# First down product of the second layer placed inside the third pair's products, with part of the first z's way back issued by ScalarE

## What is computed

```
x: 3072 x 512 (output of the first layer), w_in: 512 x 1024, w_out: 1024 x 512
h   = x @ w_in
e   = exp(h - max(h)) ;  solu = h * e / (sum(e) + 1e-9)
z   = (solu - mean(solu)) / sqrt(var(solu) + 1e-6) * g_ln
out = z @ w_out
```

## Time and profile before

| | us |
|---|---|
| median of 3 runs | 869.15 (868.05 to 872.74) |
| profiled execution | 869.12 |
| its span (first to last instruction) | 867.3 |
| outside the span | 1.82 |
| TensorE busy | 857.2 (99%) |
| VectorE / ScalarE / GpSimd busy | 449.7 (52%) / 332.3 (38%) / 241.0 (28%) |
| mean granted TensorE clock | 0.998 of full |

### The profile page before, as it was taken

One profiled execution on the slowest core, in us unless ns is written; L12 is line 12 of the kernel. 1 busy time (PEld: TensorE's weight loads), 2 busy tenths in 40 slices (PEclk: granted clock), 3 DMA queues, 4 the chain that ended last, 5 costly groups with the idle time before them and its releaser, 6 DMA issues.

```text
span 867.3 us, 12108 instructions
## 1 busy us (share of the span) xinstructions
PE 857.2 (99%) x4816; PEld 700.5 (81%) x4816; DVE 449.7 (52%) x770; ACT 332.3 (38%) x505; POOL 241.0 (28%) x228
## 2 busy tenths in 40 slices
PE   8999999999999999999999999999989999999998
PEld 7788878888888888888888788888868888888886
DVE  5545543333433333323432333567889899898831
ACT  2433342122311233112321223256456667676542
POOL 2654543222232222222222122227411111221000
PEclk9999999999999999999999999999999999999999
DMA  9921102111111111121021104300155654446451
GB/s 335 370 76 59 49 21 78 49 50 49 49 60 51 49 37 61 49 71 52 0 85 37 37 1 143 101 25 24 43 170 184 176 176 153 146 152 191 130 165 66
DMA packets 50744, 82.85 MB, mean 96 GB/s; under 512 B 5248, under 2 KB 23680, under 8 KB 50688
## 3 DMA queue, kind: packets, MB, share of 16 engines
q1 hardware_dynamic: 50688, 82.08, 29.0%
HBM read 56.90 MB, written 25.17 MB: 95 GB/s over the span
## 4 chain that ended last, share of the span: by engine, by line
PE 97%; DMA 1%; DVE 1%; SPq 1%; ACT 0%; issue 0%; DVEq 0%
PE acc L413 31%; PE h L383 29%; PE o_ps L947 15%; PE p L887 13%; PE att L320 3%; PE att L331 2%; PE att L355 1%; PE att L345 1%; DMA q<-in_q 1%; PE acc L331 0%; DMA zt<-z 0%; PE h L400 0%; SPq L219 0%; DVE x_lo L603 0%; SPq L852 0%
## 5 line engine op out<-in xcount | busy, mean ns | idle before, releaser
L413 PE MATMUL acc<-g_hi,w 128*128 128x512 f32 x768 | 257.2, 396 | 0.0
L383 PE MATMUL h<-x_hi,w 128*128 128x512 f32 x760 | 249.8, 389 | 0.5 <-DVE x_lo L603 0.5
L734 POOL TENSOR_TENSOR g_lo<-g_raw,g_hi 128x512 fp32r<-128x512 f32 x96 | 126.2, 1315 | 396.2 <-ACT g_hi L454 396.2
L506 ACT ACTIVATE g_raw<-g_raw,half_bias 128x512 f32<-128x512 f32 x96 | 69.5, 724 | 337.1 <-DVE g_raw L662 337.1
L413 PEld LDWEIGHTS acc<-g_hi,w 128*128 128x128 f32 x768 | 144.1, 188 | 35.1 <-issue 3.4
L383 PEld LDWEIGHTS h<-x_hi,w 128*128 128x128 f32 x760 | 142.7, 188 | 30.6 <-DVE x_lo L603 0.9
L662 DVE TENSOR_SCALAR g_raw<-h 128x512 f32<-128x512 f32 x96 | 66.2, 690 | 172.2 <-PE acc L413 172.2
L413 PE MATMUL acc<-g_lo,w 128*128 128x512 f32 x384 | 149.6, 390 | 0.0
L383 PE MATMUL h<-x_lo,w 128*128 128x512 f32 x380 | 147.9, 389 | 0.0
L667 DVE TENSOR_TENSOR g_raw<-h,g_raw 128x512 f32<-128x512 f32 x96 | 66.4, 692 | 69.6 <-ACT g_raw L506 69.6
L454 ACT ACTIVATE g_hi<-g_raw 128x512 fp32r<-128x512 f32 x96 | 60.7, 632 | 72.8 <-DVE g_raw L667 72.8
(11 more groups left out here) (116 smaller groups left out, 1051.9 us busy)
## 6 DMA issues: line engine op xcount, KB each, us to landing
z<-zq SPq DMA_DIRECT2D x24, 512.0 KB, 2.7
zt<-z SPq DMA_DIRECT2D x96, 128.0 KB, 3.1
kT<-in_kT SPq DMA_DIRECT2D x24, 256.0 KB, 2.7
q<-in_q SPq DMA_DIRECT2D x24, 256.0 KB, 2.6
v<-in_v SPq DMA_DIRECT2D x24, 256.0 KB, 3.0
x2T<-y SPq DMA_DIRECT2D x24, 256.0 KB, 2.6
x_raw<-x2T SPq DMA_DIRECT2D x12, 512.0 KB, 4.8
out<-o SPq DMA_DIRECT2D x24, 256.0 KB, 4.4
```

The costliest lines, as they stand in the source:

```text
L383: last = mm(hb[f % 2][:, :], ww, xx[:, kt, :], start=kt == 0 and t == 0, stop=kt == KT - 1 and t == 2)
L413: last = mm(acc[m][:, :], ww, gg[:, f % 2, :], start=f == 0 and t == 0, stop=f == FT1 - 1 and t == 2)
L506: nc.scalar.activation(gate[:, f % 2, :], gate[:, f % 2, :], ACT.Square, bias=half_bias[:, 0:1], scale=0.5).then_inc(sem["squared"], 1)
L734: tt(g[1][:, f % 2, :], gate[:, f % 2, :], g[0][:, f % 2, :].bitcast(F32), ALU.subtract)\
```

## The change

- TensorE: `down(0)` no longer follows `up(1)`. In `up(2)` the order of the products becomes 1, 4, `down(0)`, 2, 6, 7, 5, 3; the other pairs keep 1, 2, 6, 7, 4, 5, 3. The waits on `products` are counted through `done(n, product)`.
- ScalarE: `output(0)` moves from the end of round 1 to round 2, behind `split_z(2)`. In round 1, behind `copy_part(1)`, ScalarE waits for the stored first z (`zq_stored[0]`) and issues two of the four loads of `get_z(0)`.
- SyncE: `get_z(0)` issues only the first two loads. `store(0)` moves from round 2, where it was ahead of `put_z(4)`, to the end of round 2, behind `get_z(5)`.
- VectorE: `turn_squares(0, SECOND)` goes ahead of `bias(0, FIRST)`; `split_z(0)` goes behind `join_p5(1)` and `join_p3(1)`.

```diff
-    DOWNS = {1: (0,), 2: (1, 2), 3: (3, 4), 4: (5,), 5: (6, 7), 6: (8, 9), 7: (10,), 8: (11, 12), 9: (13, 14),
+    ORDER = (1, 2, 6, 7, 4, 5, 3)
+    THIRD = (1, 4, 2, 6, 7, 5, 3)
+
+    DOWNS = {2: (1, 2), 3: (3, 4), 4: (5,), 5: (6, 7), 6: (8, 9), 7: (10,), 8: (11, 12), 9: (13, 14),
              10: (15,)}
...
+        def done(n, product):
+            return 7 * n + (THIRD if n == 2 else ORDER).index(product) + 1
+
+        def quarter(s, q):
+            squares = z_dram[s % 2].rearrange("(i r) (q x) -> q r i x", r=SQ, q=P // SQ)
+            return zt[q * SQ:(q + 1) * SQ, s % 2, :, :, :].rearrange("r i f c -> r i (f c)"), squares[q]
...
-                squares = z_dram[s % 2].rearrange("(i r) (q x) -> q r i x", r=SQ, q=P // SQ)
-                for q in range(P // SQ):
-                    sp.dma_start(zt[q * SQ:(q + 1) * SQ, s % 2, :, :, :].rearrange("r i f c -> r i (f c)"),
-                                 squares[q]).then_inc(sem["zt_loaded"][s % 2], 16)
+                for q in range(2 if s == 0 else P // SQ):
+                    dst, src = quarter(s, q)
+                    sp.dma_start(dst, src).then_inc(sem["zt_loaded"][s % 2], 16)
 
             for n in range(PAIRS2 - 1):
                 if n + 2 < PAIRS2:
                     load_x2(n + 2)
-                for s in DOWNS.get(n - 1, ()):
-                    store(s)
+                if n >= 3:
+                    for s in DOWNS[n - 1]:
+                        store(s)
                 put_z(2 * n)
                 put_z(2 * n + 1)
                 get_z(2 * n)
                 get_z(2 * n + 1)
                 if n == 0:
                     finish["store_x2"]()
+                if n == 2:
+                    store(0)
...
+                def p4():
+                    wait(pe, sem["taken"], 5 * n - 1)
+                    product(bank_of(n, 4), a(1, SECOND), t(2))
...
+                def p3():
+                    pe.wait_ge(sem["taken"], 5 * n + (1 if n else 3))
+                    product(bank_of(n, 3), s(3), b(1, RIGHT))
...
+                elif n == 2:
+                    p1()
+                    p4()
+                    down(0)
+                    p2()
+                    p6()
+                    p7()
+                    p5()
+                    p3()
...
             for n in range(1, PAIRS2 - 2):
                 copy_part(n)
+                if n == 1:
+                    act.wait_ge(sem["zq_stored"][0], 16)
+                    act.wait_ge(sem["g_used"], BLOCKS * FT1 - 1)
+                    for q in range(2, P // SQ):
+                        dst, src = quarter(0, q)
+                        nc.scalar.dma_start(dst, src).then_inc(sem["zt_loaded"][0], 16)
                 split_x(n + 1)
                 split_z(2 * n - 2)
+                if n == 2:
+                    output(0)
...
-                for s in DOWNS[n]:
+                for s in DOWNS.get(n, ()):
                     output(s)
...
             variance(0, FIRST)
+            turn_squares(0, SECOND)
             bias(0, FIRST)
-            turn_squares(0, SECOND)
             finish["dve_evacuate"]()
             turn_squares(0, FIRST)
...
             join_p7(1)
             join_p4(1)
-            split_z(0)
             join_p5(1)
             join_p3(1)
+            split_z(0)
             split_x(2, True)
```

More of the change, by code:

```diff
@@ L902, in t, with p1, p2, p6 @@
                     return [lambda k, w=w: w[:, i, k, :] for w in w_sum]
+                def p1():
+                    wait(pe, sem["part_copied"], n)
+                    pe.wait_ge(sem["x2_lo"], 2 * n + 1)
+                    product(bank_of(n, 1), a(0, FIRST), b(0, LEFT))
+                def p2():
+                    wait(pe, sem["h_max"], 2 * n)
+                    product(bank_of(n, 2), a(1, FIRST), b(1, LEFT))
+                def p6():
+                    pe.wait_ge(sem["x2_lo"], 2 * n + 2)
+                    product(bank_of(n, 6), s(1), t(1))
+                def p7():
+                    product(bank_of(n, 7), s(2), b(0, RIGHT))
+                def p4():
+                    wait(pe, sem["taken"], 5 * n - 1)
+                    product(bank_of(n, 4), a(1, SECOND), t(2))
+                def p5():
+                    product(bank_of(n, 5), s(0), t(0))
+                def p3():
+                    pe.wait_ge(sem["taken"], 5 * n + (1 if n else 3))
+                    product(bank_of(n, 3), s(3), b(1, RIGHT))
                 if n == 0:
@@ L908, in up @@
                     pe.wait_ge(sem["w2_in_lo"], 7)
[L909 to L916, removed]
+                    p1()
+                    p2()
                     pe.wait_ge(sem["gmax"], BLOCKS * FT1 - 1)
-                pe.wait_ge(sem["x2_lo"], 2 * n + 2)
-                product(bank_of(n, 6), s(1), t(1))
-                if n == 0:
+                    p6()
                     pe.wait_ge(sem["part_copied"], 1)
[L922 to L925, removed]
+                    p7()
                     finish["pe_down"](FT1 - LAG - 1)
@@ L928, in up @@
                     pe.wait_ge(sem["taken"], 1)
-                if n == 1:
+                    p4()
+                    pe.wait_ge(sem["taken"], 2)
+                    p5()
+                    p3()
+                elif n == 1:
+                    pe.wait_ge(sem["h_max"], 2)
+                    p1()
+                    p2()
+                    p6()
+                    pe.wait_ge(sem["gmax"], BLOCKS * FT1)
+                    p7()
                     for par in range(2):
                         pe.wait_ge(sem["acc_free"][par], 2 * BLOCKS)
[L932 to L937, removed]
+                    p4()
+                    p5()
+                    p3()
+                elif n == 2:
+                    p1()
+                    p4()
+                    down(0)
+                    p2()
+                    p6()
+                    p7()
+                    p5()
+                    p3()
+                else:
+                    p1()
+                    p2()
+                    p6()
+                    p7()
+                    p4()
+                    p5()
+                    p3()
             def down(s):
@@ L973, in copy_part @@
             def copy_part(n):
-                act.wait_ge(sem["products"], 7 * n + 1)
+                act.wait_ge(sem["products"], done(n, 1))
                 wait(act, sem["h_max"], 2 * n)
@@ L1089, in join_p2 @@
                 dve.wait_ge(sem["part_copied"], n + 1)
-                dve.wait_ge(sem["products"], 7 * n + 2)
+                dve.wait_ge(sem["products"], done(n, 2))
                 add_with_maximum(h2[:, FIRST, LEFT], bank_of(n, 2)[:, :], part, -3.4e38, st("h_first", FIRST))\
@@ L1094, in join_p6 @@
             def join_p6(n):
-                dve.wait_ge(sem["products"], 7 * n + 3)
+                dve.wait_ge(sem["products"], done(n, 6))
                 dve.wait_ge(sem["taken"], 5 * n + 1)
@@ L1099, in join_p7 @@
             def join_p7(n):
-                dve.wait_ge(sem["products"], 7 * n + 4)
+                dve.wait_ge(sem["products"], done(n, 7))
                 dve.wait_ge(sem["taken"], 5 * n + 2)
@@ L1104, in join_p4 @@
             def join_p4(n):
-                dve.wait_ge(sem["products"], 7 * n + 5)
+                dve.wait_ge(sem["products"], done(n, 4))
                 dve.wait_ge(sem["taken"], 5 * n + 3)
@@ L1110, in join_p5 @@
             def join_p5(n):
-                dve.wait_ge(sem["products"], 7 * n + 6)
+                dve.wait_ge(sem["products"], done(n, 5))
                 dve.wait_ge(sem["taken"], 5 * n + 4)
@@ L1118, in join_p3 @@
             def join_p3(n):
-                dve.wait_ge(sem["products"], 7 * n + 7)
+                dve.wait_ge(sem["products"], done(n, 3))
                 dve.wait_ge(sem["taken"], 5 * n + 5)
```

## The result

The changed kernel takes 877.46 us (median of 6 runs, 876.06 to 880.03) against 868.96 for the kernel before (6 runs). The ratio is 1.0097, 95% interval 1.0071 to 1.0122: slower by 8.5 us, inside the range on record and 1 us above the forecast of 876.5.

The account below looks back on a forecast made before the run. TensorE was taken to bound the kernel (97% of the chain). 869.12 + 5.6 (later product 3 of pair 3) + 1.74 (clock tail) = 876.5 us; 8-in-10 range 873.0 to 879.5.

Parts of the forecast that it names:

- Part 1: Start of z's way: store out 0.25 us sooner, but product 4 of pair 1 stalls 0.5 us (0 to 0.9).
- Part 2: Two z loads issued by ScalarE: 0.6 to 1.6 us for both, pair 2's product 1 about 0.1 later.
- The loads land likely a microsecond sooner: First z's loads: no later than 635.1 as before, likely a microsecond sooner.
- Part 3: First down product, inside pair 2: starts at 637.7 after a 1.4 us wait, without a clock fall.
- Part 4: Rest of pairs 1 and 2: `down(2)` waits 1.4 us, ends at 662.5; 1.8 us gained up to pair 3's product 3.
- five products (6.80): Pair 2 after `down(0)`: five products take 6.80 us, from 643.3 to 650.1, without a pause.
- Part 5: First store behind pair 2's z loads: holds `output(2)`; pair 3's product 3 idles 7.2 us, starting 5.6 later than before.
- The clock tail: Behind the pause at pair 3's product 3: lower clock costs 1.74 us more, bounds 0 to 3.4.
- Rival (a): The first store is no obstacle and the kernel gets faster: 867.3 us, or 863.9 without new waits; chance 0.05.
- (d): Moving `down(0)` fails: z late, clock tail there too; 877 to 878 us; chance 0.74 together with the forecast.
- (c): Blocked at pair 3, and more: landing 5.6 us, double tail, `down(4)` waiting; 880.3 us; chance 0.12.
- "No cost" at `down(4)`: z's low part due at 685.3, TensorE at 686.4: margin 1.1 us, no cost, up to 1.5 if the tail is short.

Follow-up runs that it names:

- e1: The changed kernel with SyncE issuing the first output store ahead of the stores of pair 2's z again: 867.03 us, ratio 0.9974.
- e4: The kernel before with only the first output store moved behind the loads of pair 2's z: 877.95 us, ratio 1.0095.
- e3: The changed kernel, store still late, with ScalarE copying product 1 of pair 3 ahead of the held output: 877.23 us, ratio 1.0090.
- e5: e3 with ScalarE's split of x for pair 4 also put ahead of the held output: 869.25 us, ratio 1.0002.
- e2: The changed kernel with the first output store between the two groups of loads of pair 2's z: 873.96 us, ratio 1.0053.

## Why the prediction was right, step by step

- Part 1, product 4 of pair 1: forecast 0.5 us later, measured 631.60 - 2.47 - 628.76 = 0.37.
- Part 2: ScalarE's two issues took 0.98 us (forecast about 0.9, bounds 0.6 to 1.6). "The loads land likely a microsecond sooner" was wrong: the high part began at 637.68 - 2.47 = 635.21, no sooner than the earlier trace rows. It changed nothing in the sum, since VectorE's joins decided.
- Part 3: `down(0)` at 639.95 - 2.47 = 637.48 (637.7), 1.26 us idle (1.4), no fall of the clock.
- Part 4: `down(2)` at 656.72 (656.9). Its pause was 0.43 and not 1.4, because a pause of 0.50 at product 3 of pair 2, which I had not listed, had already taken part of it. The step that failed is "five products (6.80)": the last of them also waits for `join_p2`, whose turn on VectorE comes after the transposes of pair 1.
- Part 5, the mechanism of the loss, came as forecast: `store(0)` issued at 672.46 (672.1; the store of z ahead of the loads took 3.04 us and not 2.65), landed 3.3 us later (4.0, bounds 3.0 to 5.6). Product 3 of pair 3 started at 677.70 (677.9), 7.13 us idle (7.2). Against before that is +5.43 (5.6).
- The landing estimate of 2.6 us from the Trainium skill ("DMA: Bandwidth & Descriptors", section on the anatomy of one DMA) lay 0.7 below the measured 3.3, my 4.0 lay 0.7 above. That section gives its figures for DMAs issued by GpSimd, and this store is SyncE's. I also misread the trace: "the quickest such group here took 3.0 to 3.2" is wrong. The stores of 256 KB issued from 829.8 to 864.9 in the kernel before land in

```profile
DMA to landing us min/median/max: 2.0/2.0/3.5
```

  and those from 843.1 on in 2.0 each, quicker than the page's estimate. The lower bound of 3.0 was too high for an unladen store; it did no harm, since this store took 3.3.
- The clock tail is the one term that was mis-sized: 1.74 taken, 3.01 measured, inside the bounds 0 to 3.4. It makes the sum 5.43 + 3.01 = 8.44 against 7.34: the tail is 1.27 too small, product 3's delay 0.17 too large, and that is the miss of 1 us.
- Rival (a), that the store is no obstacle, fell with e1 and e4. (d) did not come: the first down product's wait stayed short. Of (c) the longer tail came in part (its sum has 3.4), its landing of 5.6 and its wait at `down(4)` did not.
- "No cost" at `down(4)` held, and by its own working: the low half of z is there at 686.89 - 2.47 + 0.65 = 685.1 (685.3), and TensorE comes to it at 687.7 (686.4, the longer tail makes up for the rest). What the forecast did not see is why: `down(4)` hangs on the same held output, and only TensorE's own pause at product 3 hides that. As soon as product 3 is freed (e3), that wait is next and as long.

## What to carry to other kernels

When a transfer is moved down an engine's list, ask who waits for its landing, what is queued behind that waiter, and what the next engine has queued behind *that*: here one store behind eight loads made ScalarE wait for the way back of a z that it had only just normalized, VectorE for ScalarE and TensorE for VectorE, and cost 10 us in a change whose own aim could win 5. A wait is priced by all that stands behind it on each engine, and freeing one item only moves the pause to the next (e3), while freeing both makes an 8 us wait cost 1.8 (e5 against e1). A step that makes something "sooner" should be tried without the others: two of them here were worth nothing or less once the real gain stood alone, by 0.3 to 0.6 us of distance, one trace each.

## What the runs showed that was not expected

The cost of the lower clock level does not follow the length of the pause before it. Pause and tail, each from one trace: 3.27 and 1.75 (e4), 3.53 and 1.74 (before), 4.67 and 2.91 (e2), 6.03 and 1.85 (e4), 7.13 and 3.01 (changed), 7.57 and 2.67 (e3). Pauses of up to 1.55 us left the clock at 1.00; the 24 matmuls behind them took 0.1 to 0.2 us longer.

Part of the reason can be read off. Granted clock in the pause of the kernel before, in that of the changed kernel, and in and behind the longer one of e4:

```profile
633.00:636.50 3.50, 0.00 (x1) 0.00 (x0) 1.07 (x4) 1.15 (x2) 0.00 (x0) 1.00 1.03 245
673.20:680.17 6.97, 0.00 (x1) 0.01 (x1) 0.70 (x2) 1.88 (x3) 0.00 (x0) 0.70 0.62 157
673.40:679.30 5.90, 0.00 (x0) 0.00 (x0) 0.64 (x2) 1.76 (x3) 0.00 (x0) 0.74 0.58 143
679.41:683.00 3.59, 3.59 (x9) 2.82 (x10) 3.54 (x5) 2.15 (x4) 0.00 (x0) 0.50 0.02 5
```

In the kernel before the clock fell only when TensorE was working again; in the two longer pauses it fell while TensorE idled, so a part of the slow stretch passed unused. What is left of it behind the pause costs about half its length: 6.13 us and a tail of 3.01 (changed), 3.59 and 1.85 (e4). So for a pause of over 3 us a tail of 1.7 to 3.0 is to be taken as a range, whatever its length; how long the lower level stays is left open.
